# Attention, routing and two expert layers on one core: GpSimd makes all four weight sums of a group in one round, and its constants and logit sums are moved

## What is computed

```
q_n, k_n = rmsnorm(q, g_q), rmsnorm(k, g_k)          # 4 batches, 12 heads, 448 rows of 64
attn = softmax(q_n @ k_n.T / 8);  o = attn @ v
x = o as 1792 rows of 768
logits = normalised x @ normalised expert_emb.T / tau; expert_idx = argmax; gate_w = softmax of it
x = gate_w * (relu(x @ w1[e]) @ w2[e])               # each row by its own one of 8 experts
out = (sigmoid(x @ w_gate) * (x @ w_val)) @ w_out    # 768 -> 1536 -> 768, for all rows
```

## Time and profile before

| what | value |
|---|---|
| median of 3 runs | 1142.76 us (1141.33 to 1145.07) |
| profiled execution | 1139.64 us |
| its span | 1138.2 us |
| PE busy | 1104.6 us, 97% |
| DVE busy | 775.7 us, 68% |
| ACT busy | 599.8 us, 53% |
| POOL busy | 367.2 us, 32% |
| DMA, mean over the span | 131 GB/s |

### The profile page before, as it was taken

The page is one execution under the profiler, slowest core; times in us unless marked ns, Lnnn a source line. Parts: engine busy times, 40 slices in busy tenths (PEclk is TensorE's granted clock), DMA queues, the critical chain, the costliest instruction groups (busy, mean ns, idle before and its releaser), DMA issues. The chain is left out here.

```text
span 1138.2 us, 22080 instructions
## 1 busy us (share of the span) xinstructions
PE 1104.6 (97%) x7392; PEld 979.2 (86%) x7393; DVE 775.7 (68%) x1411; ACT 599.8 (53%) x1415; POOL 367.2 (32%) x367
## 2 busy tenths in 40 slices
PE   8999999999889899999999899999999999999997
PEld 6666666666579899999999899999999999999997
DVE  5788878997786554665466886575579675674672
ACT  5877878777536454655465752242345343441441
POOL 7798888887520110111012403000013012000002
PEclk9999999999989999999999999999999999999999
DMA  4345664444338676777687342331331434331312
GB/s 126 104 144 147 191 205 134 138 120 133 108 89 208 177 200 161 207 205 193 165 211 204 96 137 72 86 110 56 111 99 42 118 105 153 102 105 45 112 42 97
DMA packets 207778, 149.62 MB, mean 131 GB/s; under 512 B 12446, under 2 KB 203550, under 8 KB 207718
## 3 DMA queue, kind: packets, MB, share of 16 engines
q1 hardware_dynamic: 203446, 133.79, 42.3%
q0 software_dynamic: 3568, 14.82, 4.3%
q10 hardware_dynamic: 704, 0.23, 0.1%
HBM read 128.29 MB, written 20.53 MB: 131 GB/s over the span
## 5 line engine op out<-in xcount | busy, mean ns | idle before, releaser
L2059 PE MATMUL qb<-BH,l_WH 128*128 128x448 f32 x504 | 185.4, 368 | 0.6 <-DVE quads L1868 0.6
L2060 PE MATMUL qb<-BL,l_WH 128*128 128x448 f32 x504 | 185.2, 368 | 0.0
L2061 PE MATMUL qb<-BH,l_WL 128*128 128x448 f32 x504 | 185.2, 368 | 0.0
L1764 ACT ACTIVATE l_WH<-stream 128x384 fp32r<-128x384 f32 x209 | 100.7, 515 | 127.4 <-PE ob L2082 102.4
L2000 POOL TENSOR_TENSOR quads<-quads 128x448 f32<-128x448 f32 x24 | 30.7, 1278 | 381.2 <-DVE quads L1868 381.2
L1868 DVE TENSOR_TENSOR quads<-qb,quads 128x448 f32<-128x448 f32 x168 | 100.0, 619 | 67.1 <-PE qb L2061 66.9
L1864 DVE TENSOR_TENSOR l_WL<-stream,l_WH 128x384 fp32r<-128x384 f32 x209 | 121.5, 599 | 20.4 <-ACT l_WH L1764 20.3
L817 ACT ACTIVATE PR<-sc,negmax 112x448 f32<-112x448 f32 x192 | 120.7, 642 | 16.7 <-DVE negmax L535 15.9
L1605 PE MATMUL hb<-XH,W1H 128*128 128x256 f32 (+1 forms) x384 | 111.5, 290 | 5.0 <-issue 4.0
L1605 PE MATMUL yb<-HH,W2H 128*128 128x256 f32 (+1 forms) x384 | 112.9, 294 | 0.4 <-DVE W2L L1547 0.4
L2080 PE MATMUL ob<-l_WH,GH 128*128 128x384 f32 x336 | 112.5, 335 | 0.4 <-DVE Y L1948 0.4
(11 more groups left out here) (261 smaller groups left out, 2545.6 us busy)
## 6 DMA issues: line engine op xcount, KB each, us to landing
raw<-in_moe_w_dram SPq DMA_DIRECT2D x68, 384.0 KB, 5.0
stream<-in_moe_w_dram SPq DMA_DIRECT2D x48, 512.0 KB, 4.7
stream<-w_sums SPq DMA_DIRECT2D x92, 192.0 KB, 2.4
w_sums<-Sb SPq DMA_DIRECT2D x12, 768.0 KB, 6.3
stream<-in_moe_w_out_dram SPq DMA_DIRECT2D x48, 192.0 KB, 2.4
stream<-in_moe_w_val_dram SPq DMA_DIRECT2D x36, 192.0 KB, 2.7
stream<-in_moe_w_gate_dram SPq DMA_DIRECT2D x33, 192.0 KB, 2.6
raw<-in_q_dram SPq DMA_DIRECT2D x24, 224.0 KB, 3.3
```

The lines of the kernel that those rows point to most:

```text
L2059: nc.tensor.matmul(bank, wh, bh, start=(k == 0), stop=False)
L2060: nc.tensor.matmul(bank, wh, bl, start=False, stop=False)
L2061: mm = nc.tensor.matmul(bank, wl, bh, start=False, stop=(k == 2))
```

## The change

- `weight_quarters`: all four sums of a group are made in the even round, one behind the other. The odd round has none.
- Of the 19 constants the first 11 get a function of their own, `first_constants`, which runs right behind the identity matrix, ahead of GpSimd's first 1/rms. The other 8 run as the hook after round 1 in place of round 3.
- `logits_early` becomes the hook after round 21 in place of 20, and DVE's `pick_early` that after round 22 in place of 21.

No instruction that computes is added or taken away.

```
--- before.py
+++ after.py
@@ -147,11 +147,32 @@
 
 
 CONSTS = 19
+FIRST_CONSTS = 11
+
+
+def first_constants(nc, c, r, pool):
+
+    def const(i, n):
+        i.then_inc(r.consts, 1)
+        pool.wait_ge(r.consts, n)
+    exact = dict(allow_small_or_imprecise_dtypes=True)
+    const(nc.gpsimd.iota(r.rank[:, :, :], [[0, EARLY], [-1, E]], base=E, channel_multiplier=0, **exact), 1)
+    const(nc.gpsimd.iota(r.cap[:, :], [[LINES * CHUNKS, E]], base=0, channel_multiplier=0, **exact), 2)
+    const(nc.gpsimd.memset(r.half[:, :], 0.5), 3)
+    const(nc.gpsimd.memset(r.ones[:, :], 1.0), 4)
+    const(nc.gpsimd.memset(r.tri[:, :], 1.0), 5)
+    const(nc.gpsimd.affine_select(out=r.tri[:, :], in_=r.tri[:, :], compare_op=ALU.is_ge, fill=0.0, base=0,
+                                  pattern=[[-1, P]], channel_multiplier=1), 6)
+    const(nc.gpsimd.memset(c.ones8[:, :], 1.0), 7)
+    const(nc.gpsimd.memset(r.mask_e[:, :, :], 1.0), 8)
+    const(nc.gpsimd.memset(r.mask_e[:, :, 0], 0.0), 9)
+    const(nc.gpsimd.memset(r.mask_l[:, :, :], 1.0), 10)
+    const(nc.gpsimd.memset(r.mask_l[:, :, 0], 0.0), FIRST_CONSTS)
 
 
 def constants(nc, c, r, pool):
 
-    done = [0]
+    done = [FIRST_CONSTS]
 
     def const(i):
         i.then_inc(r.consts, 1)
@@ -159,18 +180,6 @@
         pool.wait_ge(r.consts, done[0])
     exact = dict(allow_small_or_imprecise_dtypes=True)
     J = MAXJOBS
-    const(nc.gpsimd.iota(r.rank[:, :, :], [[0, EARLY], [-1, E]], base=E, channel_multiplier=0, **exact))
-    const(nc.gpsimd.iota(r.cap[:, :], [[LINES * CHUNKS, E]], base=0, channel_multiplier=0, **exact))
-    const(nc.gpsimd.memset(r.half[:, :], 0.5))
-    const(nc.gpsimd.memset(r.ones[:, :], 1.0))
-    const(nc.gpsimd.memset(r.tri[:, :], 1.0))
-    const(nc.gpsimd.affine_select(out=r.tri[:, :], in_=r.tri[:, :], compare_op=ALU.is_ge, fill=0.0, base=0,
-                                  pattern=[[-1, P]], channel_multiplier=1))
-    const(nc.gpsimd.memset(c.ones8[:, :], 1.0))
-    const(nc.gpsimd.memset(r.mask_e[:, :, :], 1.0))
-    const(nc.gpsimd.memset(r.mask_e[:, :, 0], 0.0))
-    const(nc.gpsimd.memset(r.mask_l[:, :, :], 1.0))
-    const(nc.gpsimd.memset(r.mask_l[:, :, 0], 0.0))
     const(nc.gpsimd.iota(r.lines[:, :], [[1, ROWS]], base=0, channel_multiplier=0, **exact))
     const(nc.gpsimd.iota(r.slots[:, :], [[1, SLOTS]], base=0, channel_multiplier=0, **exact))
     const(nc.gpsimd.iota(r.token[:, :].rearrange("p (b t) -> p b t", t=NT), [[S, B], [1, NT]], base=0,
@@ -456,7 +465,6 @@
                         if there(it, n - 2):
                             pool.wait_ge(c.sums_written, 16 * step)
                         first_weight_sums(nc, c, pool, 4 * step + 1)
-                    else:
                         last_weight_sums(nc, c, pool, 4 * step + 2)
 
             def step(it, n):
@@ -496,9 +504,10 @@
                     nc.gpsimd.tensor_scalar(r.HI[:, i, :], r.slots[:, :], r.a[:, i:i + 1], None,
                                             ALU.is_equal).then_inc(r.hi_e[0], 1)
 
+            first_constants(nc, c, r, pool)
             first_rms(0)
             first_rms(1)
-            pipeline(step, -2, PAIRS, pool, {-2: emb_norm, 3: lambda: constants(nc, c, r, pool), 20: logits_early})
+            pipeline(step, -2, PAIRS, pool, {-2: emb_norm, 1: lambda: constants(nc, c, r, pool), 21: logits_early})
             early_slots(POOL_SLOTS[0:EARLY // 2])
             x_squares(0, PAIRS - 2)
             pool.wait_ge(r.ssq_e, 1)
@@ -800,7 +809,7 @@
             for i in range(2):
                 dve.wait_ge(first_step, 2 * i + 2)
                 over_rms_of(nc.vector, 0, i).then_inc(first_normed, 1)
-            dve_hooks = {-1: emb_scale, 0: emb_out, 21: pick_early, PAIRS - 1: early_ranks, PAIRS: early_lines}
+            dve_hooks = {-1: emb_scale, 0: emb_out, 22: pick_early, PAIRS - 1: early_ranks, PAIRS: early_lines}
             pipeline(step, -1, PAIRS, dve, dve_hooks)
             finish()
 

```

## The result

The changed kernel takes 1152.1 us (median of 7, 1148.94 to 1155.65) against 1142.47 us (7 runs, 1139.11 to 1145.07): ratio 1.0085, 95% interval 1.0067 to 1.0102, slower by 7.7 to 11.7 us. The profiled execution took 1148.94 us, its span is 1147.4 us, 9.2 us more than before.

What follows compares the result with a forecast made beforehand. The prediction took attention to be bound by PE. Waits of 10.7 us in place of 4.04 (+6.6), less 0.4 given back, made +6.2 us on 1142.8: 1149.0 us, range 1144.5 to 1152.5.

Steps and rivals of the forecast that it cites:

- rival 3: Attention rounds: longer PE stalls put ACT and DVE out of step, +10.1 us in all, 1152.9 us; chance 0.10.
- Constants, -1.43 us: Start and round 1: moving the 19 constants removes PE's stall of 1.43 us at pair 6.
- the sign given: Start-up: with the eleven constants before 5 us, the first 1/rms starts no later.
- Logit sums: Pair 23: 3.18 us of logit sums go behind its qkn, removing the 1.81 us stall unless something else stands there.
- The four sums, 10.42 us from landing to transpose: Odd pairs: 8.51 us plus 1.91 us from first sum to PE's transpose; 10.7 us of waits for 4.04, +6.6 us.
- rival 1: First sum of even rounds: blocks come sooner, start at most 1.3 us behind PE's transpose; -4.0 us, 1138.8 us; chance 0.07.
- What PE gives back, 0.4 us: Rounds behind PE's stalls: PE regains a little behind each, 0.4 us for six more stalls.
- A stall of PE does not bring the next blocks earlier: SP's loads in attention: SP follows PE, so the stalls do not cancel each other; no size of its own.
- DVE against GpSimd, zero: DVE's denominator addition meeting POOL's work: gain at late odd pairs, loss at even pairs; zero, 1.5 us either side.
- The rival on the other side: The same as rival 1, first sum of even rounds: waits only disappear, 1138.8 us; chance 0.07.

Runs made afterwards that it cites:

- changed_again: The changed kernel measured once more without a further edit: 1157.15 us, ratio 1.0105 to the kernel before.
- no_two_port_add: The kernel before with DVE's addition of 1e-9 to the denominator replaced by a reduction over an axis of length one: 1141.91 us, ratio 0.9987.
- blocks_one_round_earlier: The changed kernel with SP writing the sums and loading the next blocks in even rounds, one round earlier: 1136.17 us, ratio 0.9943 to the kernel before.
- only_the_sums: The kernel before with only the four sums put into the even round, constants and logit sums unmoved: 1158.92 us, ratio 1.0151.

## Why the prediction was right

Forecast 1149.0 us (+6.2), range 1144.5 to 1152.5; measured 1152.1 us (+9.6) in the median, which lies in the range, near its upper end. It lies above the forecast's own range of 1146.5 to 1151.5 us, and nearer to rival 3's 1152.9 us than to the forecast. The mechanism was that of the forecast, with the clock's part on top. That the wider range held is in part luck: it had been widened for rival 3's trouble on DVE, which did not come, and the clock, which was in no term, took up that room.

- *Constants, -1.43 us:* right. The wait at pair 6 is gone. The eleven constants end at 4.2 us, and the first 1/rms starts at 6.37 us in place of 6.23. That is 0.1 us later, against the sign given, but over the eleven traces this start lies between 6.17 and 6.48 us, in either order of the constants.
- *Logit sums:* right. At pair 23 1.23 us are left of 1.81, and they are the weight sums' own, twice the 0.62 us forecast and not "well under 1 us". DVE's moved instructions cost nothing, as put: from pair 23's second transpose to the mark it was 27.58 us before (280.71 to 308.29 us) and 27.63 us after (290.91 to 318.54 us).
- *The four sums, 10.42 us from landing to transpose:* 10.43 us measured. The waits by pair, forecast and measured: pair 7 1.2 and 1.11; pair 9 1.45 and 1.93; pair 11 1.90 and 1.23; pair 13 2.71 and 2.71; pair 15 1.1 and 1.50; pair 17 0.31 and 1.06; pair 19 0.7 and 1.09; pair 21 0.7 and 0.46; pair 23 0.62 and 1.23. The sum is 12.3 us for 10.7. The distances from transpose to landing were taken from one trace, and they scatter by half a microsecond and more: in changed_again pair 15 waits 0.33 us. For pair 7 the prediction called 1.57 us the shortest distance of any round; its own trace has 1.41 us at pair 4 (49.82 to 51.23 us), which also brings rival 1's limit of 1.3 us closer than it says. The changed kernel had 2.54 us ahead of pair 7 (72.52 to 75.06 us), and from there on 1.93 us at the least, at pair 20; at pair 4 it had 1.24 us, and pair 5 has no wait. Pair 17's was short for a reason that I had in hand and did not follow: DVE's held addition of 2.99 us at 178.37 us was followed by PE waiting 0.5 us for a low half in that very round, so that its transpose of pair 16 came late and the landing looked near.
- *What PE gives back, 0.4 us:* this did not come. Behind a wait the round is 0.1 us shorter (85.51 to 97.13 us, 11.62), but the round that ends in a wait is 0.1 us longer without the wait itself (97.13 to 110.90 us less 1.93, 11.84), so the two cancel.
- *"A stall of PE does not bring the next blocks earlier":* right. SP's write of `Sb` follows pair 11's transpose by 5.69 us both times (133.60 to 139.29 us before, 137.27 to 142.96 us after). At pair 9, where the clock fell in between, it came 1.5 us later, as PE did (5.77 us before, 7.22 us after).
- *DVE against GpSimd, zero:* as forecast. The long holds are gone from the changed kernel (the longest is 1.02 us) without a gain that could be told, and no_two_port_add shows why: PE waited for one of them only, 0.5 us. The Trainium skill's rule (SBUF — State Buffer, Summary: rules for kernel authors) that the two engines block each other holds in kind here: in both kernels every addition of over 0.25 us fell on POOL's products (qkn, sq or xq), those on the power took 0.16 us, and the reduction in its place is never held. In which mode an instruction runs is in no trace, so the mode as the cause is not shown directly. In size the rule does not hold, since a hold of 2.99 us spans three of POOL's instructions of 1.0 us.
- *The clock, missing from the sum.* Rival 3 had longer waits as its cause, but spoke of ACT and DVE and not of the granted clock. 3.1 us of the 10.2 us at the mark are two falls of it. This is the term that I left out. The Trainium skill (TensorE: Matmul & The Clock Gate, HAM oscillation — how this bites in real kernels) warns that idle gaps of TensorE lower its clock. Here it fell behind gaps of 1.93 and 2.71 us; behind those of 1.43 and 1.81 us in the kernel before it had stayed at its upper level, and the prediction, which forecast a wait of 2.71 us, longer than either, put no term for it.

The rival on the other side, that the blocks come sooner, needed one more edit: blocks_one_round_earlier is that case, and it takes 0.9943 of before (forecast for it: 4 us under, 0.9965).

The account of the 10.2 us at the mark: 8.3 us more of waits for qkn, 3.1 us of clock behind pairs 9 and 13, 0.8 us more at the first normalised k (1.20 us; it was 0.37 us), 0.6 us less for the low halves, and 1.3 us less for the start-up's fall of the clock, which the trace of before has: 10.3 us.

## What to carry to other kernels

In this kernel, where POOL waits for a transfer, what stands behind the wait moved the end, and not how much POOL does per round: 1.9 us of sums per group, moved from a round with room to just behind the landing, cost 13.8 us at the mark (304.73 to 318.54 us), while with the same four sums a round later, or the blocks a round earlier, the mark stood at 302.13 and 303.48 us. Before an instruction is pulled ahead, look at what the producer of its input follows; here SP followed TensorE, so the sums could only be early if SP's turn was moved with them. And time saved on an engine that is hardly waited for (18 us of DVE) gained nothing that could be told.

## What I had not expected of the hardware

- Waits of PE at which the granted clock fell to half: 1.70, 1.71, 1.93, 1.99, 2.16, 2.71, 2.75 and 3.96 us. Waits at which it did not fall: 1.67, 1.74, 1.81, 1.88 and 1.92 us, and all shorter ones in attention's rounds. From 1.70 to 1.93 us it went either way. The fall came as late as 1.7 us behind the end of the wait (1.99 us, changed_again) and as early as 1.7 us ahead of it (3.96 us, only_the_sums). It cost 1.5 to 1.7 us where the clock was down for some 3 us, and 2.9 and 2.5 us where it was down for some 7 us (2.75 and 3.96 us, only_the_sums).
- DVE's addition over 8 elements a row took up to 2.99 us while GpSimd ran products back to back, past several of their ends; as a reduction it took 150 to 153 ns every time.
